# Block products that accumulate on banks copied in between, and the activation's slope in the first pass

## The chip, the cores and the metric

One core of a Trainium2 chip. The time is the device time of one execution in microseconds (us); of the kernel before there are three runs, with a median of 1401.9 us.

## The reference

Three layers on 4608 rows of 512 numbers: an attention block, a mixture of 8 experts, and the layer that this change is about:

```python
def _moe2_ref(x, w_in, w_out, alpha):          # x (4608, 512), w_in (512, 2048), w_out (2048, 512)
    h = x @ w_in
    g = np.maximum(h, 0.0) + alpha * np.minimum(h, 0.0)   # one alpha for each of the 2048 columns
    return (g @ w_out).astype(np.float32)
```

All is fp32. The kernel makes an fp32 product of three matmuls: each operand is split into a rounded high part and the rest, and high x high, high x low and low x high are added up.

## The kernel before

Attention and experts run until about 652 us; the change doesn't touch them. They leave the rows in DRAM. Then comes the last stage, in two passes.

**First pass** (`h = x @ w_in`, stored as `acts` in DRAM). The rows are worked in 8 groups `g` (B = 8) of 544 rows (TB = 544, two halves of TH = 272). The weights stay in SBUF; the output columns are worked in 8 blocks `c` (NP = 8), each of 128 columns in the lower half and 128 in the upper. So there are 64 blocks, numbered n = 8 g + c. Each block is a 2x2 product of halves (columns, rows, and the 512 that are summed over), and it is made with seven products instead of eight, as Winograd's form of Strassen's scheme has it. With U2 = P1 + P6 and U3 = U2 + P7 the four parts are

```
C11 = P1 + P2      C12 = U2 + P5 + P3      C21 = U3 + P4      C22 = U3 + P5
```

Here C11 and C12 go to the lower columns (h = 0 in the buffer `gb`), C21 and C22 to the upper ones (h = 1). A product is 6 matmuls of 128x272 (two halves of the sum, three matmuls each) and has a PSUM bank of its own (`ps_p`). TensorE runs them in the order P1, P2, P6, P7, P4, P5, P3 (`group`, `product`, lines 1558 to 1575), and before each it waits until the bank is free from the block before (line 1566). ScalarE copies P1 to SBUF (`copy_p1`, L897); VectorE does all sums (`add`, L1230, and one wide add for C21 and C22, L1256). SyncE stores both halves of `gb` to `acts` (`store_acts`, L524); `gb` has two buffers, and their first writers wait for the store of two blocks before (`free_acts`).

The moving operands of the seven products of a group are made from the rows `yz`, which SyncE loads in four quarters, one ahead of the stores of each of the blocks 0 to 3 of the group before (`load_y`, L518 and L519). VectorE transposes them (`turn_y`, L1206, in two parts in blocks 4 and 5), makes four sums (`sums_12`, `sums_34`, in blocks 5 and 6), ScalarE rounds the seven (`high`, L889) and VectorE makes the rests (`low`, L1224), both in block 7. The order of the instructions on each engine is written out by hand; every engine takes its own in that order.

In the last group ScalarE and VectorE also split two blocks of w_out per block (L909 and L1279), and the first tile of the second pass is prepared.

**Second pass** (`g @ w_out`), 34 tiles of 128 rows: SyncE loads a tile of `acts` (1 MB, L531), VectorE makes min(h, 0) x alpha (`negative`, L1291) and adds max(h, 0) (`rectify`, L1297), ScalarE rounds (`tile_high`, L917), VectorE makes the rest (`tile_low`, L1302), and TensorE does 48 matmuls of 128x512 (`down`). Tile 0 follows the first pass at once; the first matmul of tile 1 waits for its rest. ScalarE copies the result out (L934) and SyncE stores it.

## Time and profile before

| | us |
|---|---|
| three runs | 1401.13, 1401.9, 1403.9 |
| profiled execution | 1401.62 |
| its span | 1399.8 |
| TensorE busy | 1340.9 (96%) |
| VectorE busy | 824.1 (59%) |
| ScalarE busy | 427.2 (31%) |
| first pass | 669 to 1013.7 |
| second pass | 1013.7 to 1395.5 |

The span is the time from the first to the last instruction; what lies around it is 1.8 us. Busy shares are means over stages that differ much. In the rows below, a releaser in brackets is what ended the idle time of the engine before the instruction. The recorded end of a matmul lies behind the start of the next, since they are pipelined. A row with x2 merges two instructions, and its length runs from the start of the first to the end of the second.

### The profile page before, as it was taken

What the parts mean: (1) busy time and instruction counts of PE and PEld (TensorE: products, weight loads), DVE (VectorE), ACT (ScalarE), POOL (GpSimd) and SP (SyncE); (2) the same over time, 40 slices, a digit from 0 to 9 for tenths busy, and PEclk for the clock granted to TensorE, in tenths of its full rate; (3) what the DMA queues carried; (4) which work ended last, traced back from release to release, by engine and by line L of the source; (5) the groups of instructions that cost most, each with busy time, mean ns of one, the idle gap of its engine ahead of it and who ended that gap; (6) DMA issues with size and microseconds to landing.
All of it is one profiled execution on the core that took longest, in us unless ns stands there. A gap on an engine that the chain in (4) does not pass through costs nothing.

```text
span 1399.8 us, 22413 instructions
## 1 busy us (share of the span) xinstructions
PE 1340.9 (96%) x7807; PEld 1157.3 (83%) x7808; DVE 824.1 (59%) x1065; ACT 427.2 (31%) x625; POOL 186.7 (13%) x232
## 2 busy tenths in 40 slices
PE   8998599999979999997899999999999999999998
PEld 7887478888868888885899999999978888888886
DVE  5677552223555535255677767778875665666652
ACT  6887341111434313134121202212322222222221
POOL 5664022121222222222000000000000000000000
PEclk9999799999989999998899999999999999999999
DMA  8785262112557423452633334433444444444452
GB/s 309 264 265 177 78 240 73 45 43 76 189 176 233 154 103 130 165 159 68 216 126 131 120 135 143 138 125 124 152 122 120 118 124 125 113 112 112 112 120 53
DMA packets 180849, 195.50 MB, mean 140 GB/s; under 512 B 25296, under 2 KB 130768, under 8 KB 180176
## 3 DMA queue, kind: packets, MB, share of 16 engines
q1 hardware_dynamic: 173552, 174.61, 39.5%
q0 software_dynamic: 6112, 19.93, 4.1%
q10 hardware_dynamic: 1152, 0.56, 0.2%
q8 instruction: 16, 0.26, 0.1%
q14 instruction: 17, 0.14, 0.0%
HBM read 127.16 MB, written 67.37 MB: 139 GB/s over the span
## 4 chain that ended last, share of the span: by engine, by line
PE 92%; DVE 3%; ACT 2%; issue 1%; ACTq 0%; DVEq 0%; DMA 0%; POOL 0%; POOLq 0%
PE ps_p L365 13%; PE ps_p L367 13%; PE ps_p L366 13%; PE ps_y L365 5%; PE ps_y L367 5%; PE ps_y L366 5%; PE ps_h L365 5%; PE ps_h L367 5%; PE ps_h L366 5%; PE ps_o L365 5%; PE ps_o L366 5%; PE ps_o L367 5%; PE ps_hT L1511 2%; PE ps_sr L1389 2%; PE ps_xT L1505 1%
## 5 line engine op out<-in xcount | busy, mean ns | idle before, releaser
L365 PE MATMUL ps_p<-b_hi,w_hi 128*128 128x272 f32 x896 | 259.6, 290 | 3.5 <-DVE b_lo L1224 3.5
L366 PE MATMUL ps_p<-b_lo,w_hi 128*128 128x272 f32 x896 | 259.8, 290 | 0.0
L367 PE MATMUL ps_p<-b_hi,w_lo 128*128 128x272 f32 x896 | 259.7, 290 | 0.0
L365 PEld LDWEIGHTS ps_p<-b_hi,w_hi 128*128 128x128 f32 x896 | 169.9, 190 | 4.4 <-DVE b_lo L1224 4.4
L367 PEld LDWEIGHTS ps_p<-b_hi,w_lo 128*128 128x128 f32 x896 | 170.1, 190 | 0.0
L366 PEld LDWEIGHTS ps_p<-b_lo,w_hi 128*128 128x128 f32 x896 | 169.5, 189 | 0.0
L365 PE MATMUL ps_h<-w_hi,xgT_hi 128*128 128x512 f32 x296 | 121.9, 412 | 9.6 <-DVE w_lo L953 7.7
L1144 DVE COPY hid<-ps_h 128x512 f32<-128x512 f32 x74 | 51.1, 691 | 135.6 <-PE ps_h L367 129.4
L365 PE MATMUL ps_y<-w_hi,hidT_hi 128*128 128x512 f32 x296 | 122.7, 414 | 0.0
L1146 DVE SCALAR_TENSOR_TENSOR hidT_lo<-ps_hT,hidT_hi 128x512 fp32r<-128x512 f32 x74 | 51.1, 691 | 121.2 <-ACT hidT_hi L829 119.6
L829 ACT ACTIVATE hidT_hi<-ps_hT 128x512 fp32r<-128x512 f32 x74 | 44.2, 598 | 245.5 <-PE ps_hT L1511 245.5
L367 PE MATMUL ps_h<-w_hi,xgT_lo 128*128 128x512 f32 x296 | 118.0, 399 | 0.0
L1291 DVE SCALAR_TENSOR_TENSOR neg<-gt,alpha 128x2048 f32<-128x2048 f32 x33 | 75.6, 2291 | 71.5 <-DMA gt<-acts 71.5
L366 PE MATMUL ps_h<-w_lo,xgT_hi 128*128 128x512 f32 x296 | 117.7, 398 | 0.0
L367 PE MATMUL ps_y<-w_hi,hidT_lo 128*128 128x512 f32 x296 | 116.5, 394 | 0.0
L1302 DVE TENSOR_TENSOR g_lo<-gt,g_hi 128x2048 fp32r<-128x2048 f32 x34 | 77.9, 2292 | 65.5 <-ACT g_hi L917 65.5
L366 PE MATMUL ps_y<-w_lo,hidT_hi 128*128 128x512 f32 x296 | 116.3, 393 | 0.0
L365 PE MATMUL ps_p<-w_hi,g_hi 128*128 128x512 f32 x272 | 107.5, 395 | 1.3 <-issue 1.3
L367 PE MATMUL ps_o<-w_hi,g_lo 128*128 128x512 f32 x272 | 107.4, 395 | 0.0
L366 PE MATMUL ps_o<-w_lo,g_hi 128*128 128x512 f32 x272 | 107.4, 395 | 0.0
L365 PE MATMUL ps_o<-w_hi,g_hi 128*128 128x512 f32 x272 | 107.4, 395 | 0.0
L366 PE MATMUL ps_p<-w_lo,g_hi 128*128 128x512 f32 x272 | 107.4, 395 | 0.0
(219 smaller groups left out, 2411.6 us busy)
## 6 DMA issues: line engine op xcount, KB each, us to landing
acts<-gb SPq DMA_DIRECT2D x128, 272.0 KB, 2.1
stage<-in_moe_w SPq DMA_DIRECT2D x32, 1024.0 KB, 5.4
gt<-acts SPq DMA_DIRECT2D x32, 1024.0 KB, 6.1
xs_all<-in_xT SPq DMA_DIRECT2D x8, 1024.0 KB, 6.4
xN_all<-in_xN SPq DMA_DIRECT2D x8, 1024.0 KB, 6.3
rows_x<-xrow SPq DMA_DIRECT2D x32, 256.0 KB, 2.6
out_rows<-orow SPq DMA_DIRECT2D x32, 256.0 KB, 2.0
yz<-rows_y SPq DMA_DIRECT2D x30, 256.0 KB, 3.1
```

Of the source, the lines that this page charges most:

```text
L365: pe.matmul(out, s_hi, m_hi, start=start, stop=False)
L366: pe.matmul(out, s_hi, m_lo, start=False, stop=False)
L367: return pe.matmul(out, s_lo, m_hi, start=False, stop=stop)
L829: act.activation(hidT_hi[:, c, :, :], ps_hT[c][:], ACT.Relu).then_inc(hT_hi_ready, 1)
L1144: dve.tensor_copy(hid[:, c, :], ps_h[c][:]).then_inc(h_copied, 1)
L1146: dve.scalar_tensor_tensor(out=hidT_lo[:, c, :, :], in0=ps_hT[c][:], scalar=0.0, in1=hidT_hi[:, c, :, :].bitcast(F32), op0=ALU.max, op1=AL ...
L1291: dve.scalar_tensor_tensor(out=neg[:], in0=gt[k % 2][:], scalar=0.0, in1=alpha[:].unsqueeze(2).to_broadcast([P, KFF, P]), op0=ALU.min, op1 ...
L1302: dve.tensor_tensor(g_lo[k % 2][:], gt[k % 2][:], g_hi[k % 2][:].bitcast(F32), ALU.subtract)\
L1389: mm = pe.matmul(ps_sr[0:NS, h * D:(h + 1) * D], a2T[:, h // GH, cc, (h % GH) * NS:(h % GH + 1) * NS], xN[par][:, cc, h * D:(h + 1) * D], ...
L1505: mm = pe.transpose(ps_xT[:, k, :], xg[:, k * P:(k + 1) * P], ident[:])
L1511: mm = pe.transpose(ps_hT[c][:, k, :], hid[:, c, k * P:(k + 1) * P], ident[:])
```

## The change

The seven products get three pairs of banks by the parity of the block. P1 goes to `ps_a`; when ScalarE has copied it out, P6 is accumulated on the same bank, which then holds U2; that is copied, P7 is accumulated (U3), that is copied, and P4 is accumulated (C21), which ScalarE copies to `gb`. P5 goes to `ps_c`; VectorE makes C22 of it and the copy of U3, then P3 is accumulated on it, and VectorE makes C12 of it and the copy of U2. P2 goes to `ps_b`. TensorE's order is P6, P5, the next block's P2, P7, the next block's P1, P4, P3, and it waits for p1_copied ahead of P6, u2_copied ahead of P7, u3_copied ahead of P4, and c22_ready ahead of P3.

The slope moves from the second pass to the first. h with a slope is h + (1 - alpha) x relu(-h): ScalarE writes relu(-h) of one half of `gb` (128x544) to the one buffer `below`, VectorE multiplies by 1 - alpha (a scalar per partition) and adds to `gb`; first h = 1, then h = 0. The stores wait for that. The second pass rounds the loaded tile directly. The transposes move from blocks 4 and 5 to blocks 2 and 3, the sums to 4 and 5, and ScalarE's roundings are spread over blocks 6 and 7. `load_y` and its place stay. The diff, cut to its core (renamed semaphores, the second pass's arguments and the removed functions are left out):

```diff
@@ order of the products, and of their blocks in w_in (SLOT; b_of is permuted to match)
-P1, P2, P6, P7, P4, P5, P3 = range(7)
+P2, P1, P6, P5, P7, P4, P3 = range(7)
@@ tensors: neg_first and neg_ go; one [P, TB] buffer comes
-        neg_first = sb("neg_first", [P, KFF, P], c=under)
+        below = sb("below", [P, TB], c=under)
-        neg_ = sb("neg", [P, KFF, P], c=sd)
-        ps_pp = pb("ps_p", [P, 7, DM], c=pd)
-        ps_p = [ps_pp[:, i, 0:TH] for i in range(7)]
-        ps_o = [pb("ps_o0", [P, DM], c=pd)[:], ps_pp[:, P1, :]]
+        ps_a = [pb(f"ps_a{i}", [P, DM], c=pd)[:, 0:TH] for i in range(2)]
+        ps_b = [pb(f"ps_b{i}", [P, DM], c=pd)[:, 0:TH] for i in range(2)]
+        ps_c = [pb(f"ps_c{i}", [P, DM], c=pd)[:, 0:TH] for i in range(2)]
+        ps_o = [pb(f"ps_o{i}", [P, DM], c=pd)[:] for i in range(2)]
@@ SyncE, store_acts
-                    wait_apart(sp, (c12_ready, c22_ready)[h], g * NP + c + 1)
+                    wait_apart(sp, acts_ready[h], g * NP + c + 1)
@@ ScalarE
+            def negative(g, c, h):
+                n = NP * g + c
+                act.wait_ge((c12_ready, c22_ready)[h], n + 1)
+                if h:
+                    act.wait_ge(c21_copied, n + 1)
+                    if not (isinstance(n, int) and n == 0):
+                        act.wait_ge(acts_ready[0], n)
+                else:
+                    act.wait_ge(acts_ready[1], n + 1)
+                act.activation(below[:], gb[c % 2][:, h, :], ACT.Relu, scale=-1.0).then_inc(below_ready[h], 1)
+
             def group(g, last=False):
                 for c in range(NP):
-                    copy_p1(g, c)
-                    if c == NP - 1 and not last:
-                        for product in range(7):
-                            high(g + 1, product)
+                    n, par = NP * g + c, c % 2
+                    again = not (isinstance(n, int) and n == 0)
+                    ahead = c >= NP - 2 and not last
+                    act.wait_ge(product_ready[P6], n + 1)
+                    if again:
+                        act.wait_ge(c12_ready, n)
+                    act.activation(part[1][:], ps_a[par], ACT.Copy).then_inc(u2_copied, 1)
+                    if ahead and c == NP - 1:
+                        high(g + 1, P6)
+                        high(g + 1, P5)
+                    act.wait_ge(product_ready[P7], n + 1)
+                    if again:
+                        act.wait_ge(c22_ready, n)
+                    act.activation(part[2][:], ps_a[par], ACT.Copy).then_inc(u3_copied, 1)
+                    if c < NP - 1:
+                        copy_p1(g, c + 1)
+                    elif not last:
+                        copy_p1(g + 1, 0)
+                    act.wait_ge(product_ready[P4], n + 1)
+                    free_acts(act, 1, NP // 2 * g + c // 2, par)
+                    act.activation(gb[par][:, 1, 0:TH], ps_a[par], ACT.Copy).then_inc(c21_copied, 1)
+                    if ahead and c == NP - 2:
+                        high(g + 1, P2)
+                        high(g + 1, P1)
+                    if ahead and c == NP - 1:
+                        high(g + 1, P7)
+                        high(g + 1, P4)
+                    negative(g, c, 1)
+                    negative(g, c, 0)
+                    if ahead and c == NP - 1:
+                        high(g + 1, P3)
                     if last:
                         act.wait_ge(wo_loaded, 64)
-                        act.wait_ge(product_ready[P4], NP * g + c + 1)
                         for f in (c, NP + c):
                             act.activation(w_out(w_hi, f), raw_out(f), ACT.Copy).then_inc(wo_hi_ready, 1)
-                        if c == 5:
-                            tile_high(0, 0)
+                        if c == 6:
+                            tile_high(0, 0, 1)
...
             for product in range(7):
                 high(0, product)
+            copy_p1(0, 0)
@@ VectorE (the adds U2, U3 and the wide C21/C22 go, with negative and rectify)
+            def c11(g, c):
+                free_acts(dve, 0, NP // 2 * g + c // 2, c % 2)
+                add(gb[c % 2][:, 0, 0:TH], ps_b[c % 2], P2, NP * g + c, part[0], p1_copied, c11_ready)
+
+            def slope(g, c, h):
+                dve.wait_ge(below_ready[h], NP * g + c + 1)
+                if h == 0:
+                    dve.wait_ge(c11_ready, NP * g + c + 1)
+                dve.scalar_tensor_tensor(out=gb[c % 2][:, h, :], in0=below[:], scalar=alpha[:, h * NP + c:h * NP + c + 1],
+                                         in1=gb[c % 2][:, h, :], op0=ALU.mult, op1=ALU.add).then_inc(acts_ready[h], 1)
+
             def group(g, last=False):
                 for c in range(NP):
                     n, par = NP * g + c, c % 2
                     ahead = c == NP - 1 and not last
+                    if c == NP - 1 and not last:
+                        low(g + 1, P2)
+                        low(g + 1, P1)
                     if ahead:
                         low(g + 1, P6)
+                    free_acts(dve, 1, NP // 2 * g + c // 2, par)
+                    add(gb[par][:, 1, TH:TB], ps_c[par], P5, n, part[2], u3_copied, c22_ready)
+                    if ahead:
+                        low(g + 1, P5)
+                    if c < NP - 1:
+                        c11(g, c + 1)
+                    elif not last:
+                        c11(g + 1, 0)
+                    add(gb[par][:, 0, TH:TB], ps_c[par], P3, n, part[1], u2_copied, c12_ready)
                     if ahead:
                         low(g + 1, P7)
                         low(g + 1, P4)
+                    slope(g, c, 1)
+                    slope(g, c, 0)
                     if not last:
+                        if c == 2:
+                            turn_y(g + 1, 0, 9)
+                        if c == 3:
+                            turn_y(g + 1, 9, 17)
                         if c == 4:
-                            turn_y(g + 1, 0, 9)
+                            sums_12(g + 1)
                         if c == 5:
-                            turn_y(g + 1, 9, 17)
-                            sums_12(g + 1)
-                        if c == 6:
                             sums_34(g + 1)
+                        if ahead:
+                            low(g + 1, P3)
...
+            dve.tensor_scalar(alpha[:], alpha[:], -1.0, 1.0, ALU.mult, ALU.add).then_inc(beta_ready, 1)
@@ TensorE
+            banks = {P1: ps_a, P2: ps_b, P6: ps_a, P5: ps_c, P7: ps_a, P4: ps_a, P3: ps_c}
...
+                fresh = p in (P1, P2, P5)
                 for k in range(2):
+                    out, m_hi, m_lo = banks[p][c % 2], b_hi[p][:, k, :], b_lo[p][:, k, :]
...
+                    pe.matmul(out, s_hi, m_hi, start=fresh and k == 0, stop=False, skip_group_check=more)
...
+            def first(g, c):
+                free(c21_copied, NP * g + c - 1)
+                product(P1, g, c)
+
+            def second(g, c):
+                free(c11_ready, NP * g + c - 1)
+                product(P2, g, c)
+
+            def group(g, last=False):
                 for c in range(NP):
-                    for p in range(7):
-                        product(p, g, c)
+                    n = NP * g + c
+                    pe.wait_ge(p1_copied, n + 1)
+                    product(P6, g, c)
+                    free(c12_ready, n - 1)
+                    product(P5, g, c)
+                    if c < NP - 1:
+                        second(g, c + 1)
+                    elif not last:
+                        second(g + 1, 0)
+                    pe.wait_ge(u2_copied, n + 1)
+                    product(P7, g, c)
+                    if c < NP - 1:
+                        first(g, c + 1)
+                    elif not last:
+                        first(g + 1, 0)
+                    pe.wait_ge(u3_copied, n + 1)
+                    product(P4, g, c)
+                    pe.wait_ge(c22_ready, n + 1)
+                    product(P3, g, c)
...
+            second(0, 0)
+            first(0, 0)
             group(0)
-            with pe.Fori(1, B) as g:
+            with pe.Fori(1, B - 1) as g:
                 group(g)
+            group(B - 1, last=True)
             down(0, 0, fresh=True)
-            pe.wait_ge(p1_copied, B * NP)
```

## Rows read from the trace of the kernel before

**Rows 1.** Busy time by stretch: PE, PEld, DVE, ACT, POOL, then clock, DMA, GB/s.

```profile
800.00:900.00 100.00, 100.00 (x798) 100.00 (x797) 74.73 (x147) 18.78 (x37) 0.00 (x0) 1.00 0.39 134
...
1100.00:1200.00 100.00, 100.00 (x430) 80.36 (x429) 61.88 (x27) 23.45 (x18) 0.00 (x0) 1.00 0.42 115
```

**Rows 2.** Timeline (start, length, instruction, idle before): the eviction behind P5, two blocks.

```profile
864.71 0.72 DVE L1256 TENSOR_TENSOR gb<-ps_p,part 128x544 f32<-128x544 f32 x1 [1.07 <-PE ps_p L367]
...
869.99 0.72 DVE L1256 TENSOR_TENSOR gb<-ps_p,part 128x544 f32<-128x544 f32 x1 [1.07 <-PE ps_p L367]
```

**Rows 3.** Timeline where P1 and P2 end; 866.68 is P6's first matmul.

```profile
866.12 0.40 ACT L897 ACTIVATE part<-ps_p 128x272 f32<-128x272 f32 x1 [4.88 <-PE ps_p L367]
...
866.68 0.29 PE L365 MATMUL ps_p<-b_hi,w_hi 128*128 128x272 f32 x1
...
866.95 0.44 DVE L1230 TENSOR_TENSOR gb<-ps_p,part 128x272 f32<-128x272 f32 x1 [0.69 <-PE ps_p L367]
```

**Rows 4.** Timeline of the first wait of TensorE in the first pass.

```profile
671.00 0.66 ACT L889 ACTIVATE b_hi<-yz 128x544 fp32r<-128x544 f32 x1 [2.56 <-DVE yz L1215]
...
671.69 0.72 DVE L1224 TENSOR_TENSOR b_lo<-yz,b_hi 128x544 fp32r<-128x544 f32 x1 [0.72 <-ACT b_hi L889]
...
672.47 0.39 PE L365 MATMUL ps_p<-b_hi,w_hi 128*128 128x272 f32 x1 [1.72 <-DVE b_lo L1224]
...
672.70 0.29 PE L366 MATMUL ps_p<-b_lo,w_hi 128*128 128x272 f32 x1
```

**Rows 5.** Timeline of ScalarE and VectorE where instructions follow in a row.

```profile
924.49 1.20 ACT L889 ACTIVATE b_hi<-yT 128x544 fp32r<-128x544 f32 x2
...
925.67 0.43 DVE L1230 TENSOR_TENSOR gb<-ps_p,part 128x272 f32<-128x272 f32 x1
926.02 0.43 DVE L1230 TENSOR_TENSOR part<-ps_p,part 128x272 f32<-128x272 f32 x1
...
929.25 1.34 DVE L1224 TENSOR_TENSOR b_lo<-yz,b_hi 128x544 fp32r<-128x544 f32 x2
...
985.35 1.16 ACT L909 ACTIVATE w_hi<-stage 128x512 fp32r<-128x512 f32 x2 [2.67 <-PE ps_p L367]
...
1002.70 1.92 ACT L917 ACTIVATE g_hi<-gt 128x2048 fp32r<-128x2048 f32 x1 [0.34 <-DVE gt L1297]
1004.52 0.37 ACT L897 ACTIVATE part<-ps_p 128x272 f32<-128x272 f32 x1
```

**Rows 6.** Groups of VectorE instructions: count, busy us, mean ns, idle before.

```profile
L992 DVE TENSOR_SCALAR a<-a,cinv 128x512 f32<-128x512 f32 x16 | 12.0, 791 | 0.3
...
L1279 DVE TENSOR_TENSOR w_lo<-stage,w_hi 128x512 fp32r<-128x512 f32 x14 | 9.0, 682 | 0.0
```

**Rows 7.** Timeline of the pass's first block: P7's start, ScalarE's copy, the pace's return.

```profile
674.55 0.60 PE L365 MATMUL ps_p<-b_hi,w_hi 128*128 128x272 f32 x1 [1.07 <-DVE b_lo L1224]
...
675.37 0.37 ACT L897 ACTIVATE part<-ps_p 128x272 f32<-128x272 f32 x1
...
680.61 0.33 PE L367 MATMUL ps_p<-b_hi,w_lo 128*128 128x272 f32 x1
```

**Rows 8.** Timeline around a y load, its line's landing, and a transpose.

```profile
860.54 0.44 DVE L1230 TENSOR_TENSOR gb<-ps_p,gb 128x272 f32<-128x272 f32 x1
...
862.29 0.41 SPq L519 DMA_DIRECT2D yz<-rows_y  x1
...
DMA to landing us min/median/max: 2.7/2.8/5.5
...
913.70 1.37 DVE L1206 STREAM_TRANSPOSE yT<-yz 128x1152 f32<-128x1152 f32 x1
```

**Rows 9.** Timeline where the second pass goes from tile 0 to tile 1.

```profile
1023.30 2.30 DVE L1302 TENSOR_TENSOR g_lo<-gt,g_hi 128x2048 fp32r<-128x2048 f32 x1 [2.04 <-ACT g_hi L917]
...
1025.70 0.47 PE L365 MATMUL ps_p<-w_hi,g_hi 128*128 128x512 f32 x1 [1.32 <-issue]
```

**Rows 10.** TensorE's busy time and granted clock in a stretch of the attention stage.

```profile
148.00:150.00 2.00, 1.30 (x11) 1.00 0.53 168
```

More of the change, by code:

```diff
@@ L52 @@
 TH = TB // 2
[L53 to L54 removed]
+P2, P1, P6, P5, P7, P4, P3 = range(7)
+SLOT = (1, 0, 4, 5, 2, 3, 6)
 XE = GH * D + E
@@ L1317, in _ @@
             group(B - 1, last=True)
[L1318 to L1324 removed]
+            tile_low(1, 1)
+            with dve.Fori(0, B) as g:
                 for k in range(4):
[L1326 to L1328 removed]
+                    tile_low(4 * g + k + 2, k)
         @block.tensor
```

109 lines of the change are left out of this document (34 added, 75 removed).

## The prediction

> **What bounds the kernel now.** I read the stretches by stage first. In the last stage's first pass (about 669 to 1013.6 us) TensorE is busy 100% of a stretch at clock 1.00, VectorE 75% and ScalarE 19% [rows 1]; the second pass shows TensorE at 100% as well, VectorE at 62%. Then I read the timeline of one block: the eviction that waits for P5 recurs every 5.28 us [rows 2]. A block is 7 products of 6 matmuls, so a product takes 0.754 us and a matmul starts each 0.1257 us, with no hole between products. So no wait is late in the steady state, and faster evictions can't shorten either pass. What is not TensorE at full pace is little: two holes at the start of the pass with a half-rate stretch behind them [rows 7], and one hole between tiles 0 and 1 of the second pass [rows 9].
>
> **Hand-overs, from rows.** ScalarE starts a copy 0.20 us after the next product has begun (P2 began one product before 866.68, at 865.92; the copy starts 866.12) and takes 0.40 us; VectorE starts 0.27 us after (866.95 against 866.68) [rows 3]. A late wait costs TensorE 0.06 us of hop (672.41 to 672.47) and 0.10 us of refill (the second matmul comes 0.23 instead of 0.126 us later) [rows 4]: a product is late by release + 0.16 us minus its due start. On ScalarE a queued instruction starts 0.10 us before the recorded end of the one ahead (1004.52 against 1002.70 + 1.92); two of 128x544 take 1.20 us, so 0.65 us one and 0.55 us each in a row. On VectorE an add takes 0.44 us and 0.35 us in a row; two of 128x544 take 1.34 us, so 0.71 us one and 0.64 us in a row [rows 5]. A hop between the two engines is 0.03 us (671.00 + 0.66 to 671.69) [rows 4].
>
> The new slope has a per-partition scalar, which no 128x544 row shows. Bounds: 0.71 us [rows 5], and 0.11 us more, which L992 (0.791 us, such a scalar) has over a plain 128x512 (0.682) [rows 5, 6]: 0.82 us. I take 0.78 us (0.70 in a row).
>
> **The change, part by part.** I set time 0 at the start of P6 of a block. The new order puts P6 at 0, P5 at 0.75, the next block's P2 at 1.51, P7 at 2.26, the next P1 at 3.02, P4 at 3.77, P3 at 4.52, and the next P6 at 5.28. Matmuls and their operands are unchanged in number and shape, so by themselves they cost nothing more.
>
> (a) *Short chain in every block.* P3 of the block before ends at 0: its add starts 0.27, slope h=1 0.62 to 1.40, ScalarE's negative h=0 (it waits for that slope, since there is one `below`) 1.43 to 2.09. The copy of P6's sum is queued behind it: 1.98 to 2.35, though P6 was finished at 0.75. P7 can start at 2.51 instead of 2.26: 0.25 us late (0.19 with the short slope, 0.29 with the long). P4's wait on the copy of P7's sum is late by 0.60 + 0.16 - 0.75 = 0.01 us; P3's wait for its bank has 0.2 us to spare. Six blocks of each of the first seven groups pay it: 42 x 0.25 = 10.5, and 63 x 0.01 = 0.6. **11.1 us.**
>
> (b) *turn_y moves from block 4 to block 2.* The SyncE queue, which the change leaves as it is, issues the last quarter of the next y in the step of block 3, behind both stores of block 2, and these now wait for the slopes. Slope h=0 of block 2 ends at 2.12 + 0.78 = 2.90. From such a release to the issue of the last load takes 1.31 us (add ends 860.98, issue 862.29), and landing 2.8 us [rows 8]: 7.01. VectorE stands in turn_y until then, transposes (1.37 us, the next can start 1.29 later, by the overlap of rows 5) [rows 8], and only then makes C22 of block 3: 8.33 to 8.77. P3 of block 3 starts at 8.93 instead of 4.78: 4.15 us, 7 groups. Before, two blocks lay between. **29.1 us.**
>
> (c) *P2 of the next group is issued inside block 7*, due at 1.51, and needs its b_lo. ScalarE rounds P2 and P1 in block 6, between the copy of C21 and the negatives: copy -0.55, rounds -0.25 and 0.30, negative 0.85 to 1.51; slope 1.54 to 2.32; negative h=0 2.35 to 3.01; slope h=0 3.04; low P2 on VectorE behind it 3.74 to 4.45. P2 starts 4.61: 3.10 us late, 7 groups. Before, the lows stood ahead of adds that had a block of slack. **21.7 us.**
>
> (d) *Block 0 of the next group.* In block 7 ScalarE rounds P7 and P4 ahead of the negatives and P3 behind, VectorE has lows P7 and P4 ahead of the slopes: add 0.27, lows 0.62 and 1.26, slope 1.90 to 2.68, negative 2.71, round P3 3.26, copy 3.81 to 4.18, P7 at 4.34 instead of 2.26: 2.08 us, 7 groups. **14.6 us.**
>
> (e) *Last group.* Two rounds of w_out (1.16 us the pair, so 0.53 us each in the queue [rows 5]) stand between the negative and the next copy: 0.25 + 1.06 = 1.31 us, six times. Before the last block comes also the first tile's g_hi (1.92, 1.82 in the queue [rows 5]), and no P2 of a next block fills in: 1.31 + 1.82 + 0.75 = 3.88; no P1 covers the wait of P4: 0.76. **12.5 us.**
>
> (f) *Start.* P6 waits for p1_copied, which ScalarE makes after all seven rounds: before, that copy ran 675.37 to 675.74 [rows 7], so P6 starts near 675.8, 5.2 us after P2 and P1. Before, P6 started 672.47 and P7 674.55: the second product ended near 670.60 (the hole before 672.47 less the tail of a matmul), so 1.87 and 1.22 us were lost, and a refill. **+2.0 us.** The half rate after it is paid in both.
>
> (g) *Slopes out of the second pass.* It takes two passes over each of 34 tiles off VectorE, work that lies beside a TensorE without a hole [rows 1], so it is worth nothing, but for one place: tile 1 waits for g_lo until 1025.60, where its turn was 1.3 us earlier, and a refill follows [rows 9]. **-1.6 us.**
>
> Sum of (a) to (g): +89.4 us, with the short slope about 85, with the long 92 (every chain above has one or two slopes).
>
> (h) *Clock.* After holes of 1.72 [rows 4] and 1.07 us, 0.9 us of work between them, 26 matmuls took from 674.55 to 680.61, 0.23 us each where 0.126 is the pace: the clock was at its lower level, 1.2 instead of 2.4 GHz, for 6.1 us [rows 7]. With TensorE 65% busy over 2 us the granted clock stayed 1.00 [rows 10]. That cost 6.06 - 26 x 0.126 = 2.8 us, 2.7 without the refill; 0.2 of it hides a wait of (a). The hole of (b) is longer than those two together: 7 x 2.5 = 17.5. That of (c), 3.1 us, I take at two thirds of that: 12; the last group's 3.9 + 0.8 once: 2.5. That of (d) at nothing. **+32 us**, between 0 and about 60 (three falls per group, 22 x 2.7).
>
> The profiled execution took 1401.6 us (the median of the runs is 1401.9, so it stands for them). 1401.6 + 89.4 + 32 = 1523.0.
>
> The Trainium skill, "TensorE: Matmul & The Clock Gate", section "HAM oscillation", has it that a wait of TensorE long enough to count as idle brings the half clock back each time, and that the work behind it starts cold. Here the start of the pass agrees. By that rule each of (b), (c) and the last group falls every time, for about 37 us instead of 32. The same page, section "A second HAM failure mode", tells of short idles between groups of matmuls on cycled PSUM banks that make the clock swing; that would be the sixth case below.
>
> **The rivals.**
> 1. No fall of the clock: 1401.6 + 89 = 1491 (1484 to 1496). For it: no row shows one hole of 4 us between stretches of dense work. Against it: two smaller holes sufficed. 0.15.
> 2. One of the long waits is covered after all (the y wait, if the loads land or are issued sooner, -29 and its clock; or the lows): 1523 - 29 - 17 = 1477 (1455 to 1482). 0.12.
> 3. More holes than I count: the h=0 bank of gb is free only when the store of two blocks ago has landed (2.0 to 5.8 us), and VectorE's C11 waits for it ahead of the chain of (a), with some 0.3 us to spare; and the clock falls at (d) too. 1545 to 1590. 0.10.
> 4. The group ends are covered and only (a), (e) and (f) stay: 1401.6 + 11.1 + 12.5 + 2.0 - 1.6 = 1426. 0.04.
> 5. Not slower: the copies are in time in every block, so every product starts when due (this decides at 0.16 us ahead of its start). Then only tile 1's gain is left: 1401.6 - 1.6 = 1400. For it: steady work of both engines fits a block (VectorE 2.4 us of 5.28). Against it: the add of P3 is followed by three dependent instructions and a copy, 2.35 us, in a gap of 2.1. 0.03.
> 6. The short holes of (a) alone keep the clock down: 2688 matmuls x 0.1 us = 270, with (a) and parts of the group ends hidden behind slower blocks: about 1690. Against it: the stretch of rows 10. 0.01.
>
> **How the numbers follow.** The forecast has the rest, 0.55: 1523. The range takes in rival 1 and half of 2, and the lower part of 3: 1470 to 1558. A measurement of this kernel tells about 0.2% from no change; all cases but 5 lie beyond it on the slow side: slower 0.97, the same 0.015, faster 0.015.
>
> **What would show it.** P3 of block 3 waiting about 4 us for C22, with VectorE idle before the transpose until the y load lands; P2 at each group's end waiting about 3 us for b_lo; P7 waiting 0.2 to 0.3 us for the copy in other blocks and 2 us in block 0; steady blocks of 5.54 us; the second pass at the old pitch without its hole; PEclk under 1 in the first pass. I am wrong if blocks last 5.28 us, if the transposes start without a wait, or if the time beyond the holes is not at half clock.

## The result and the profile after

The changed kernel takes 1535.1 us (median of 4 runs, 1531.4 to 1536.4), the kernel before 1401.8 us on the same chip: 1.0942 times as long, 95% interval 1.0927 to 1.0957. The forecast was 1523.0, in a range of 1470 to 1558. The profiled execution took 1536.4 us with a span of 1534.6.

By the starts of the matmuls, the first pass begins at 673.4 us (before: 669.0), the second at 1149.2 (1013.0), and the span ends at 1534.6 (1399.8). So of the 134.8 us more, 4.4 come ahead of the pass, 131.8 in it, and the second pass is 1.4 shorter.

Busy time by stretch in the changed kernel answers to [rows 1]; the columns are the same. The first line is most of the first pass, the second lies in the second pass.

```profile
740.00:1140.00 400.00, 333.08 (x2305) 321.04 (x2304) 217.77 (x367) 182.07 (x385) 0.00 (x0) 0.91 0.28 99
1200.00:1300.00 100.00, 100.00 (x430) 80.36 (x429) 20.51 (x9) 22.43 (x18) 0.00 (x0) 1.00 0.43 116
```

TensorE stands idle for 67 of these 400 us, and the granted clock (1.00 is full speed, 0.50 half) is 0.91 on average. VectorE, 75% busy before, is busy 54% of the time here although two slopes per block were added: it waits as well. The second pass is full as before, with VectorE at 21% instead of 62%, and no faster for it. The new operations, from the page's groups of instructions (they answer to [rows 6]):

```profile
L1283 DVE SCALAR_TENSOR_TENSOR gb<-below,alpha,gb 128x544 f32<-128x544 f32 x128 | 100.2, 783 | 57.3 <-ACT below L911 56.9
L911 ACT ACTIVATE below<-gb 128x544 f32<-128x544 f32 x128 | 84.1, 657 | 103.6 <-DVE gb L1283 75.3
```

Who waited for whom in the first pass: engine, line, releaser, us in all, times, the longest. TensorE's three long lines are the copy of U2 ahead of P7 (`ps_a`), C22 ahead of P3 (`ps_c`) and a rest (`b_lo`) ahead of P2 (`ps_b`). The list counts a wait from the recorded end of the matmul ahead, which lies behind the next one's turn, so it misses short ones: by the starts of the matmuls P7 is late 49 times and by 37.9 us in sum.

```profile
DVE gb L1283 <- ACT below L911: 56.9, 71, 1.0
...
DVE gb L1272 <- DMA acts<-gb: 32.7, 33, 2.4
...
DVE yT L1247 <- DMA yz<-rows_y: 30.0, 7, 4.5
...
PE ps_a L1596 <- ACT part L921: 28.7, 27, 3.7
...
PE ps_c L1596 <- DVE gb L1272: 28.0, 7, 4.2
...
PE ps_b L1596 <- DVE b_lo L1265: 21.5, 8, 3.0
```

The chains themselves, from the timeline (start, length, instruction, idle before). First block 3 of a group: the transpose waits for the load of y, C22 follows it, and P3 (the last line) follows C22.

```profile
826.84 1.38 DVE L1247 STREAM_TRANSPOSE yT<-yz 128x1152 f32<-128x1152 f32 x1 [4.31 <-DMA yz<-rows_y]
828.14 0.40 DVE L1272 TENSOR_TENSOR gb<-ps_c,part 128x272 f32<-128x272 f32 x1
...
828.60 0.59 PE L1596 MATMUL ps_c<-b_hi,w_hi 128*128 128x272 f32 x1 [4.03 <-DVE gb L1272]
```

Then block 7 and the next block 0. The slope at 792.50 stands ahead of the rest that P2 needs, and P2 starts at 793.97. At 803.67 P7 of block 0 starts, 0.51 us after the start of the copy of P6's sum.

```profile
792.50 0.78 DVE L1283 SCALAR_TENSOR_TENSOR gb<-below,alpha,gb 128x544 f32<-128x544 f32 x1 [0.78 <-ACT below L911]
...
793.20 1.35 DVE L1265 TENSOR_TENSOR b_lo<-yT,b_hi 128x544 fp32r<-128x544 f32 x2
...
793.97 0.40 PE L1596 MATMUL ps_b<-b_hi,w_hi 128*128 128x272 f32 x1 [2.97 <-DVE b_lo L1265]
...
803.16 0.38 ACT L921 ACTIVATE part<-ps_a 128x272 f32<-128x272 f32 x1
...
803.67 0.39 PE L1596 MATMUL ps_a<-b_hi,w_hi 128*128 128x272 f32 x1 [1.90 <-ACT part L921]
```

And the short chain of an ordinary block: add C12, slope, `below`, the copy, and P7 at 754.91 where 754.66 was its turn (P2 began at 753.91).

```profile
752.70 0.43 DVE L1272 TENSOR_TENSOR gb<-ps_c,part 128x272 f32<-128x272 f32 x1
753.04 0.78 DVE L1283 SCALAR_TENSOR_TENSOR gb<-below,alpha,gb 128x544 f32<-128x544 f32 x1
753.91 0.66 ACT L911 ACTIVATE below<-gb 128x544 f32<-128x544 f32 x1 [0.92 <-DVE gb L1283]
...
754.48 0.38 ACT L921 ACTIVATE part<-ps_a 128x272 f32<-128x272 f32 x1
...
754.91 0.40 PE L1596 MATMUL ps_a<-b_hi,w_hi 128*128 128x272 f32 x1
```

The clock, in stretches of 2 us around the holes of P2 (793.97) and P7 (803.67); a hole is a time in which TensorE waits, and the last column but two is the granted clock. Behind each of these two holes some 3.4 us are at the lower level of 1.2 GHz.

```profile
792.00:794.00 2.00, 0.03 (x1) 0.03 (x1) 1.50 (x3) 1.84 (x4) 0.00 (x0) 1.00 0.35 139
794.00:796.00 2.00, 2.00 (x11) 2.00 (x12) 1.19 (x2) 0.00 (x0) 0.00 (x0) 0.63 0.37 139
796.00:798.00 2.00, 2.00 (x11) 2.00 (x11) 0.79 (x2) 0.40 (x1) 0.00 (x0) 0.52 0.00 0
...
804.00:806.00 2.00, 2.00 (x14) 2.00 (x13) 0.61 (x2) 0.47 (x2) 0.00 (x0) 0.69 0.39 142
806.00:808.00 2.00, 2.00 (x11) 2.00 (x11) 0.44 (x1) 0.86 (x3) 0.00 (x0) 0.50 0.48 136
808.00:810.00 2.00, 2.00 (x17) 2.00 (x17) 1.13 (x2) 0.78 (x2) 0.00 (x0) 0.96 0.00 0
```

The pace shows it directly. Matmuls start 0.23 us apart from 804.77 to 808.17, and 0.13 us apart from there on, so 15 of them took 3.4 us where 1.9 was due: 1.5 us lost.

```profile
807.95 0.39 PE L1597 MATMUL ps_c<-b_lo,w_hi 128*128 128x272 f32 x1
808.17 0.29 PE L1598 MATMUL ps_c<-b_hi,w_lo 128*128 128x272 f32 x1
808.30 0.29 PE L1596 MATMUL ps_a<-b_hi,w_hi 128*128 128x272 f32 x1
```

### The profile page after: what moved, and what is told of

It reads as the page before. It is cut to its first block, busy times and chain, and to the rows that moved or that the text cites. A ratio compares the mean times of both kernels' runs of the same rounds, so it can differ in the third digit from the quotient of the medians.

```text
span 1534.6 us, 22819 instructions
## 1 busy us (share of the span) xinstructions
PE 1396.6 (91%) x7807; PEld 1198.3 (78%) x7808; DVE 673.3 (44%) x934; ACT 570.7 (37%) x945; POOL 186.7 (12%) x232
## 4 chain that ended last, share of the span: by engine, by line
PE 76%; DVE 9%; ACT 6%; issue 4%; DMA 4%; SPq 1%; ACTq 1%; DVEq 0%; POOL 0%; POOLq 0%
PE ps_o L367 8%; PE ps_o L368 8%; PE ps_o L369 8%; PE ps_h L367 4%; PE ps_y L367 4%; PE ps_y L369 4%; PE ps_y L368 4%; PE ps_h L369 4%; PE ps_h L368 4%; DVE gb L1283 4%; PE ps_a L1596 3%; PE ps_a L1598 3%; PE ps_a L1597 3%; DMA acts<-gb 2%; PE ps_hT L1537 2%
## 5 line engine op out<-in xcount | busy, mean ns | idle before, releaser
L367 PE MATMUL ps_o<-w_hi,g_hi 128*128 128x512 f32 x544 | 215.0, 395 | 0.0
L368 PE MATMUL ps_o<-w_lo,g_hi 128*128 128x512 f32 x544 | 214.9, 395 | 0.0
L369 PE MATMUL ps_o<-w_hi,g_lo 128*128 128x512 f32 x544 | 214.9, 395 | 0.0
L1596 PE MATMUL ps_a<-b_hi,w_hi 128*128 128x272 f32 x512 | 163.3, 319 | 35.6 <-ACT part L921 28.7
L1598 PE MATMUL ps_a<-b_hi,w_lo 128*128 128x272 f32 x512 | 157.6, 308 | 0.0
L1597 PE MATMUL ps_a<-b_lo,w_hi 128*128 128x272 f32 x512 | 157.5, 308 | 0.0
L1596 PEld LDWEIGHTS ps_a<-b_hi,w_hi 128*128 128x128 f32 x512 | 106.7, 208 | 46.9 <-ACT part L921 28.1
L367 PEld LDWEIGHTS ps_o<-w_hi,g_hi 128*128 128x128 f32 x544 | 102.1, 188 | 25.0
L368 PEld LDWEIGHTS ps_o<-w_lo,g_hi 128*128 128x128 f32 x544 | 102.1, 188 | 24.8
L369 PEld LDWEIGHTS ps_o<-w_hi,g_lo 128*128 128x128 f32 x544 | 102.0, 187 | 25.0
```

The lines of the kernel that those rows point to most:

```text
L367: pe.matmul(out, s_hi, m_hi, start=start, stop=False)
L368: pe.matmul(out, s_hi, m_lo, start=False, stop=False)
L369: return pe.matmul(out, s_lo, m_hi, start=False, stop=stop)
L1596: pe.matmul(out, s_hi, m_hi, start=fresh and k == 0, stop=False, skip_group_check=more)
L1597: pe.matmul(out, s_hi, m_lo, start=False, stop=False, skip_group_check=more)
L1598: mm = pe.matmul(out, s_lo, m_hi, start=False, stop=k == 1, skip_group_check=more)
```

## The experiments

| kernel | what it is | us | ratio to before, 95% interval |
|---|---|---|---|
| e1 | transposes back in blocks 4 and 5 | 1505.1 | 1.0703 to 1.0739 |
| e2 | y loaded in blocks 0 and 1 | 1489.7 | 1.0585 to 1.0631 |
| e3 | copy of U2 ahead of `below` h = 0 | 1508.4 | 1.0724 to 1.0761 |
| e4 | rests P2 and P1 in block 6 | 1509.0 | 1.0738 to 1.0777 |
| e5 | e2 + e3 + e4, roundings earlier | 1450.6 | 1.0327 to 1.0361 |
| e6 | e5 + first copy of P1 early | 1444.5 | 1.0286 to 1.0314 |
| e7 | e2 without any slope | 1406.7 | 1.0011 to 1.0035 |
| e8 | kernel before + slopes | 1462.4 | 1.0412 to 1.0448 |
| e9 | e6, C11 behind the slopes | 1441.0 | 1.0253 to 1.0285 |
| e10 | e9, work for the next group spread | 1436.2 | 1.0221 to 1.0249 |
| e11 | e10, last group eased | 1433.0 | 1.0202 to 1.0230 |
| e12 | e11, VectorE's extra work behind C22 | 1418.7 | 1.0089 to 1.0123 |

The kernel before took 1403.6 to 1404.0 us beside them. e1 to e4 each take one or two terms of the prediction's sum away. "Late" below is what a product's first matmul starts behind its turn.

**e1.** The y wait, from the side of the transposes:

```diff
-                        if c == 2:
+                        if c == 4:
                             turn_y(g + 1, 0, 9)
-                        if c == 3:
+                        if c == 5:
                             turn_y(g + 1, 9, 17)
```

(with `sums_12` and `sums_34` one block later, too)

> The changed kernel with the transposes and sums back in the blocks where they stood before the change (4 and 5, sums in 5 and 6). Theory (separate holes, each with its own cause): the hole of about 4.2 us before P3 of block 3 goes in 7 groups, with its half-clock stretch (1.35 us each and twice 2.4 to 2.6): 7 x 4.2 + 12 = 41 us off; but block 5 now has a transpose of 1.15 us and two sums of 1.4 us behind the slopes, which end at 2.8 of a block, so C22 of block 6 is made at 5.3 instead of 3.85 and P3 of block 6 is about 1.1 us late: 8 us back. 1535 - 33 = 1502 us. Rival (the y load is not what VectorE waits for, or the time comes back at the next wait in line): less than 10 us off, 1525 or more.

Measured 1505.1, 30 us less. No transpose waits for a load any more. P3 still waits for C22 seven times, now in block 6, 1.2 us late each time, since the rest of the transposes and the sums stand ahead of C22 there.

**e2.** The same wait, from the side of the load:

```diff
-                    if c < QB:
-                        load_y(g + 1, (c,))
+                    if c < 2:
+                        load_y(g + 1, (2 * c, 2 * c + 1))
```

> The changed kernel, its transposes left in blocks 2 and 3, but SyncE issues two quarters of y ahead of the stores of block 0 and two ahead of those of block 1, so that the last one doesn't stand behind the stores of block 2. Theory: the hole before P3 of block 3 goes and nothing takes its place: 1535 - 41 = 1494 us. Some us back are possible where a store is late behind two more loads. Rival (the place of the transpose in VectorE's order is the cause, not the load): no gain, 1530 or more.

Measured 1489.7, 45.4 less. P3's line is gone from the list of waits, and 12 half-rate stretches are left of 22. Both edits remove the hole of (b), by different ways. Its price was 29.8 us of holes and 12.3 us at half rate behind them (see below). e1 gets these 42 us back and pays 9 of them again at P3 of block 6 and some 3 at P2 and P7. e2 pays nothing at P3, since its transposes in blocks 2 and 3 find C22 in time, and the half rate came behind only three of its seven holes of (d).

**e3.** The short chain of (a) and (d):

```diff
                     negative(g, c, 1)
+                    if c < NP - 1:
+                        copy_u2(g, c + 1)
+                    elif not last:
+                        copy_u2(g + 1, 0)
                     negative(g, c, 0)
```

> The changed kernel, with ScalarE's copy of U2 of the next block ahead of the negative of h=0 instead of behind it. Theory: this takes the slope of h=1 and the negative out of the way of P7. The waits of P7 in ordinary blocks go (42 x 0.34 = 14 us), the 2.15 us in block 0 of each group with its half-clock stretch (7 x 3.3 = 23 us), and 1.3 us in six blocks of the last group (8 us): 1535 - 45 = 1490 us. P2's 3.1 us and P3's 4.2 us stay. Rival (the copy-and-accumulate chain itself is too long for a block, whatever stands in ScalarE's queue): P7 waits as before, less than 10 us off.

Measured 1508.4, above what was expected. Most of P7's waits went, but P3 waited more. The wait list of e3:

```profile
PE ps_c L1604 <- DVE gb L1280: 38.1, 12, 5.4
...
DVE yT L1255 <- DMA yz<-rows_y: 29.6, 7, 4.4
```

Twelve times and 38.1 us instead of seven and 28.0. TensorE comes to P3 of block 3 sooner, but y doesn't land sooner, so part of the time that (a) and (d) gave back was spent there: this P3 is 5.2 to 5.5 us late instead of 4.0 to 4.4, 8 us more in seven groups. The rest of the 18 us between expected and measured is mostly new short waits: P4 eleven times, 8.5 us in sum (0.8 before the edit), and P3 in other blocks, 5.7 us.

**e4.** The rests ahead of P2:

```diff
-                    if c == NP - 1 and not last:
-                        low(g + 1, P2)
-                        low(g + 1, P1)
...
                     add(gb[par][:, 0, TH:TB], ps_c[par], P3, n, part[1], u2_copied, c12_ready)
+                    if c == NP - 2 and not last:
+                        low(g + 1, P2)
+                        low(g + 1, P1)
```

> The changed kernel, with VectorE's two rests for P2 and P1 of the next group in block 6 ahead of the slopes instead of in block 7. Theory: b_lo of P2 is there at about 1.5 of block 7, so P2's wait of 3.1 us goes; the slopes of block 6 come 1.3 us later, and P7 of block 7, hidden behind P2's hole until now, is 1.5 us late: 7 x 1.6 us off, and some of the half-clock stretches behind P2's hole (1.25 us each): 1535 - 11 - 6 = 1518 us. Rival (P2 waits for something else): no change.

Measured 1509.0, 26 less, where 17 were expected. P2's wait is gone; P7's grew from 28.7 to 36.2 us in sum, since the slopes of block 6 now come later (P7 of block 7 is 1.4 us late, as expected). The 9 us beyond the expectation are in part the clock's: the half rate costs 12 us less than in the changed kernel, not 6, for it came behind only four of the seven holes of (d). The profiled execution also began the pass 4 us earlier.

**e5.** The three together, and the roundings P6, P5 and P3 earlier (`copy_u2` as in e3, loads as in e2, rests as in e4):

```diff
+                    if ahead and c == NP - 2:
+                        high(g + 1, P6)
+                        high(g + 1, P5)
                     if ahead and c == NP - 1:
                         high(g + 1, P3)
+                    negative(g, c, 0)
```

> The changed kernel with all holes between blocks taken on at once: y loads issued in blocks 0 and 1, the copy of U2 ahead of the negative of h=0, the rests of P2 and P1 in block 6, and ScalarE's roundings of P6, P5 (block 6) and P3 (block 7) put between the copy of U2 and that negative, where ScalarE would wait for VectorE's slope. Banks, accumulation and slopes are as changed. Theory (accumulating on copied banks costs nothing by itself; all of the loss was queue order): left are the start (+2 us), the last group (about 4 us before the last block and the first tile) and crumbs of 0.1 us in some blocks (5 us), less 1.6 us for tile 1: 1401.8 + 2 + 4 + 5 - 1.6 = 1411 us. Rival (the chain of product, copy, product is too tight, since P4 has no time to spare, and slips in every block): 64 x 0.3 us or more, 1430 us.

Measured 1450.6, 40 us above the theory. The rival's time fits, its mechanism doesn't: P4 is late in 11 of the 64 blocks, not in every one (10.0 us in sum, 3.2 of it in the last block). Two half-rate stretches are left, at the pass's start and end, so the clock's part is nearly gone. What remains are waits that the longer ones had covered, above all P3's: 43 times, 22.6 us late in sum. The wait list of e5:

```profile
DVE gb L1280 <- DMA acts<-gb: 78.7, 62, 2.5
...
PE ps_c L1604 <- DVE gb L1280: 16.5, 30, 1.0
```

C11 waits in 62 of 64 blocks until the store of two blocks ago has landed, and C12 and the slopes are queued behind it.

**e6.** The start:

```diff
             for product in range(7):
                 high(0, product)
-            copy_p1(0, 0)
+                if product == P1:
+                    copy_p1(0, 0)
```

> As e5_waits_out, and ScalarE copies P1 of the very first block right after it has rounded P1, instead of after all seven. Theory: P6 no longer waits 5.3 us at the start, only for its own b_lo (1.9 us), and P5 and P2 of the next block fill in before P7: 3 us less than e5_waits_out, and no half-clock stretch there (2 us): 1406 us, between the kernel before and e5_waits_out. Rival (the products at the start wait for their b_lo one after the other anyway): the same as e5_waits_out within 1 us.

Measured 1444.5, 6.1 less where 5 were expected. The hole ahead of P6 shrank from 5.3 to 2.0 us, and the half-rate stretch behind it from 21 slow matmuls to 14, 0.8 us less. By the starts of the matmuls the pass is 3.7 us shorter (390.7 to 387.0); the rest of the 6.2 us between the two profiled executions lies ahead of the pass, which began 2.5 us earlier and varies in all kernels (see below).

**e7.** What the accumulation on copied banks costs alone. This is e2 with `below` and the slopes left out altogether, so negative numbers of h pass unchanged; stores wait for the adds and copies:

```diff
-                    wait_apart(sp, acts_ready[h], g * NP + c + 1)
+                    wait_apart(sp, (c12_ready, c22_ready)[h], g * NP + c + 1)
+                    if h:
+                        wait_apart(sp, c21_copied, g * NP + c + 1)
+                    else:
+                        wait_apart(sp, c11_ready, g * NP + c + 1)
...
-                    negative(g, c, 1)
-                    negative(g, c, 0)
...
-                    slope(g, c, 1)
-                    slope(g, c, 0)
```

> The changed kernel with y loads in blocks 0 and 1 and with the activation's slope left out altogether (neither the negatives nor the multiply-adds; the second pass rounds h itself). The copies, the accumulation on the banks and the queue order are as changed. Theory: without slopes no wait of a block is late; left are the start (+2 us), 2.5 us before the last block, less 1.6 us: about 1405 us. Rival (the accumulation on copied banks is what costs): P7's and P4's waits stay, 1440 us or more.

Measured 1406.7. The wait list of e7, TensorE's lines in the first pass with the hole of the start and two small ones:

```profile
PE ps_a L1596 <- ACT part L903: 5.1, 1, 5.1
...
PE ps_a L1596 <- ACT part L925: 1.2, 1, 1.2
...
PE ps_b L1596 <- DVE b_lo L1267: 0.7, 1, 0.7
```

So the four times per block that TensorE goes on with a bank which another engine has read in between (P6, P7, P4 and P3) cost it nothing in the steady state. Beside e2, which has the same loads, the slopes cost 83 of its 86 us. No run without slopes has the loads of the changed kernel; that the wait for y hangs on the slopes too, through the stores that wait for them, is argued and not shown.

**e8.** The other half alone: the kernel before, with both slopes at the end of each block, the stores waiting for them, and the second pass without the activation:

```diff
-                    wait_apart(sp, (c12_ready, c22_ready)[h], g * NP + c + 1)
+                    wait_apart(sp, acts_ready[h], g * NP + c + 1)
...
                     add(gb[par][:, 0, TH:TB], P3, n, gb[par][:, 0, TH:TB], c12_ready)
+                    slope(g, c, 1)
+                    slope(g, c, 0)
```

> The kernel before (seven banks, its own order of products and its sums on VectorE), with only the slope moved into the first pass as the change has it (ScalarE's negative, VectorE's multiply-add, stores behind them). Theory: banks have a block of slack, so no chain is late, but VectorE has about 9.7 us free in a group of 42.2 and the slopes want 16 x 0.70 = 11.2: TensorE slips 1.5 us in each of 7 groups and some 4 us in the last, less 1.6 us: 1415 us. Rival (a hidden engine stays hidden): 1400 us. Other rival (the slopes cost TensorE as much as in the changed kernel): 1480 us or more.

Measured 1462.4, 47 above my sum. VectorE in two blocks of e8:

```profile
792.00 0.78 DVE L1249 SCALAR_TENSOR_TENSOR gb<-below,alpha,gb 128x544 f32<-128x544 f32 x1
793.57 0.79 DVE L1249 SCALAR_TENSOR_TENSOR gb<-below,alpha,gb 128x544 f32<-128x544 f32 x1 [0.79 <-ACT below L908]
794.27 0.44 DVE L1243 TENSOR_TENSOR gb<-ps_p,part 128x272 f32<-128x272 f32 x1
...
796.67 0.44 DVE L1243 TENSOR_TENSOR gb<-ps_p,gb 128x272 f32<-128x272 f32 x1
797.03 0.78 DVE L1249 SCALAR_TENSOR_TENSOR gb<-below,alpha,gb 128x544 f32<-128x544 f32 x1
```

The block repeats after 5.03 us (792.00 to 797.03) and VectorE waits only for `below`, 0.79 us between the two slopes; my sum of busy times had left that out. Eight such blocks and the work for the next group take 49.5 us a group by the repeat of the groups, where TensorE needs 42.2. With VectorE doing all seven sums, the slope makes it the bound. In the changed kernel the banks and ScalarE have taken over some of the sums (VectorE is 54% busy in the stretch above), and e12 below shows that what is left is nearly all order.

**e9.** Against the store wait of e5:

```diff
-                    if c < NP - 1:
-                        c11(g, c + 1)
-                    elif not last:
-                        c11(g + 1, 0)
                     add(gb[par][:, 0, TH:TB], ps_c[par], P3, n, part[1], u2_copied, c12_ready)
...
                     slope(g, c, 0)
+                    if c < NP - 1:
+                        c11(g, c + 1)
+                    elif not last:
+                        c11(g + 1, 0)
```

> e6_start_too with one move: VectorE makes C11 of the next block behind both slopes instead of ahead of C12, so that its wait for the landed store of two blocks ago no longer holds up C12. Theory (what e5 and e6 still lose is that wait: it takes about 2.5 us from a slope's end to the landed store, and C12, both slopes and ScalarE's negative stand behind it): VectorE's waits for that store go, P3 and P7 are in time in ordinary blocks, and about 1.3 us stay late in blocks 7 and 0 of each group, where C11 now stands ahead of C22 and of rests: 1401.8 + 20 + 4 - 1.6 = 1424 us. Rival (VectorE has too little time for its work in a block, whatever the order): no gain, 1440 us or more.

Measured 1441.0, only 3.5 under e6. The line of the store wait is gone from the list, and P3's wait rose from 16.5 us in e5 to this:

```profile
PE ps_c L1605 <- DVE gb L1281: 20.7, 42, 0.9
```

The store wait was real but not what decided, and the 1424 us expected were missed by 17. P4's waits fell (9.7 us late in e6, 3.0 here), but P3 is now late 49 times, 29.4 us in sum, in the blocks 0 and 3 to 7: C22 came late for another reason. The time is the rival's (1440 or more), but its reason, too little time on VectorE, is refuted by e12, which does the same work in 1418.7. Those short waits had no fall of the clock behind them, as this stretch of e9 shows (columns as before):

```profile
700.00:1000.00 300.00, 282.39 (x2162) 273.54 (x2160) 197.67 (x341) 169.68 (x354) 0.00 (x0) 1.00 0.33 117
```

**e10.** Two things spread over blocks 6 and 7 instead of in a heap: ScalarE's roundings, and VectorE's rests and C11 of the next group ahead of C12 of block 7:

```diff
+                    if ahead and c == NP - 2:
+                        high(g + 1, P2)
...
+                    if ahead and c == NP - 1:
+                        high(g + 1, P7)
...
+                    if ahead:
+                        c11(g + 1, 0)
+                        low(g + 1, P7)
```

> e9_c11_behind with the work for the next group spread so that each piece stands in a gap: ScalarE rounds P2 before the copy of U3 and P1 before the copy of C21 of block 6, P6 ahead of and P5 behind the negative of h=0, P7 behind the copy of U3 and P4 behind C21 in block 7; VectorE makes the rests of P2 and P1 ahead of C12 of block 6 and C11 of the next group ahead of C12 of block 7. Theory: block 6 to 7 without a wait, about 0.5 us late in block 0 (7 x 0.5), 5 us in the last group, start 1.5 us better than in the kernel before, less 1.6 us: 1401.8 + 3.5 + 5 - 1.5 - 1.6 = 1407 us. Rival (crumbs of refills and copies add up to 0.2 us a block): 1418 us.

Measured 1436.2, above both the theory (1407) and the rival (1418). Only blocks 1 and 2 of a group are free of waits. VectorE there, C12 at 783.21 and again at 788.48, which is 5.27 us and the old period:

```profile
783.21 0.44 DVE L1284 TENSOR_TENSOR gb<-ps_c,part 128x272 f32<-128x272 f32 x1 [1.29 <-PE ps_c L1610]
...
785.90 0.43 DVE L1284 TENSOR_TENSOR gb<-ps_b,part 128x272 f32<-128x272 f32 x1
786.74 0.44 DVE L1284 TENSOR_TENSOR gb<-ps_c,part 128x272 f32<-128x272 f32 x1 [0.41 <-ACT part L930]
788.48 0.44 DVE L1284 TENSOR_TENSOR gb<-ps_c,part 128x272 f32<-128x272 f32 x1 [1.29 <-PE ps_c L1610]
...
793.35 0.40 PE L1608 MATMUL ps_c<-b_hi,w_hi 128*128 128x272 f32 x1 [0.40 <-DVE gb L1284]
```

The last line is P3 of block 3, in which a transpose stood ahead of C22. By its start it is 0.6 us late, and P3 of the blocks 0 and 3 to 7, where rests, transposes or sums stand ahead of C22, is late by 0.1 to 0.7 us in the first seven groups: with the last group, 49 times and 21.1 us in sum. In the bracket of 788.48 lies what points to e12: VectorE is idle for 1.29 us between C22 and C12. It waits there in 50 of the 64 blocks, and has only 0.41 ahead of C22.

**e11.** The last group: a block of w_out less in block 5, where the first tile is rounded instead:

```diff
-                        if c == 6:
+                        if c == 5:
                             tile_high(0, 0, 1)
+                        else:
+                            round_out(c if c < 5 else c - 1)
```

> e10_spread with the last group eased: the first tile's high part is made in block 5 in place of two rounds of w_out, which move one block on each (the last pair behind the group), and its rest behind C22 of the last block. Theory: the 3.9 us before P7 and P3 of the last block become 0.6 + 0.8, and the second pass starts about 1 us late: 2 us less than e10_spread, 1405 us. Rival (the second pass waits for the moved w_out parts): 1 to 3 us more than e10_spread.

(the rest of that tile moves behind C22 of block 7)

Measured 1433.0, 3.2 under e10. In e10 the rounding of the first tile in front of the last block's copies still made P4 3.0 and P3 1.3 us late, with a half-rate stretch behind; here they are 1.3 and 0.5 us late, P4 of the block before is 0.5, and that stretch is gone.

**e12.** VectorE's transposes, sums and rests of w_out go into that gap, and so does the rest for P6, which stood ahead of C22 (those for P5, P2 and P1 were in the gap already). The rest for P7 moves behind C12 and that for P4 between the slopes; P3's stays at the block's end:

```diff
+                        if 1 <= c < 6:
+                            rest_out(c - 1)
+                        if c == 7:
+                            tile_low(0, 0)
                     add(gb[par][:, 0, TH:TB], ps_c[par], P3, n, part[1], u2_copied, c12_ready)
+                    if ahead:
+                        low(g + 1, P7)
                     slope(g, c, 1)
+                    if ahead:
+                        low(g + 1, P4)
                     slope(g, c, 0)
                     if c < NP - 1:
                         c11(g, c + 1)
+                    if ahead:
+                        low(g + 1, P3)
```

(the transposes and sums stand unchanged, but now ahead of `add(... P3 ...)`, as the first lines do)

> This is e11 with VectorE's transposes of y, its sums, its last roundings (P4, P3, P2, P1) and the rests of w_out in the gap that VectorE has between C22 and C12, instead of ahead of C22; the rounding P4 stands between the two slopes, and C11 of the next group behind C22 of block 7. Theory: what is left in e11 is order ahead of C22 alone, 0.36 to 0.67 us in each of blocks 3 to 6 of seven groups (some 15 us) and some 2.6 us of the last group. Then the median is about 1412 to 1418 us, with some 0.5 us a group left in block 0, the start and the last block. Rival: the work only moves the wait, to P7 (which then waits for C12 or for the slope behind it) or to the next P3: 1428 us and more. Neither expects it below the kernel before.

Measured 1418.7, 14.3 under e11 and 1.0106 of before: most of the theory's drop, just above the 1418 at the upper edge of what was expected. In the first seven groups there is no wait left in blocks 1 to 7 (in the last one P4 waits twice, 0.5 and 1.3 us). One is left at the group's turn, and it is longer than the 0.5 us expected:

```profile
757.91 0.43 DVE L1289 TENSOR_TENSOR gb<-ps_b,part 128x272 f32<-128x272 f32 x1
...
760.47 0.44 DVE L1289 TENSOR_TENSOR gb<-ps_b,part 128x272 f32<-128x272 f32 x1 [1.55 <-DMA acts<-gb]
760.83 1.35 DVE L1282 TENSOR_TENSOR b_lo<-yz,b_hi 128x544 fp32r<-128x544 f32 x2
761.60 0.40 PE L1618 MATMUL ps_a<-b_hi,w_hi 128*128 128x272 f32 x1 [1.43 <-DVE b_lo L1282]
```

C11 of the next group waits for the store of two blocks ago, the rest for P6 stands behind it, and P6 starts 1.6 us late. With its refill (the 0.10 us by which the second matmul comes late) and 0.34 us at the P3 that follows, this comes to 2.0 us in each of seven groups, 14.0 in all, about the whole distance of the first pass from that of the kernel before (358.8 against 344.0 us). To put that rest ahead of C11 is the next edit. It wasn't tried, and if it gave all of this back it would reach the kernel before, not pass it.

## Why the prediction was right

All steps stood but one part of (h): that the hole of (d) has no fall of the clock behind it. Their sizes come from the starts of all 2688 matmuls of the pass in the profiled execution. The pitch is the 0.1257 us from one start to the next; a step is what a product starts late, with the refill of 0.10 us, and (h) is what the matmuls behind lose by a slower pace. The start, (f) and its clock, is the difference to the kernel before.

| step | predicted, us | measured, us |
|---|---|---|
| (a) P7 of ordinary blocks | 11.1 | 15.8 |
| (b) P3 of block 3, y load | 29.1 | 29.8 |
| (c) P2 of the next group | 21.7 | 22.7 |
| (d) P7 of block 0 | 14.6 | 15.0 |
| (e) last group | 12.5 | 13.0 |
| (f) start | 2.0 | 2.1 |
| (g) second pass | -1.6 | -1.4 |
| (h) clock | 32 | 33.3 |
| begin of the pass | 0 | 4.4 |

The measured column sums to 134.7 of the 134.8. Of the 12 us between the forecast of 1523.0 and the median of 1535.1, (a) and the begin of the pass are the most, 4.7 and 4.4.

- **(a)** was mis-sized. Of its 42 waits three are 1.3 to 1.7 us, at which C11 had waited for a store ahead of the chain (rival 3's mechanism, 4.5 us here). Of the others, the seven in block 4 are covered by the hole of (b) and the slow matmuls behind it, and 32 cost 0.35 us on average instead of 0.25. The hop from the slope to `below` is 0.09 us (753.04 + 0.78 to 753.91), where I had 0.03 from [rows 4], and in the chain shown above the copy of P6's sum ends 2.45 us after P6's start at 752.41, where I had 2.35. Blocks with such a wait and nothing else mostly last 5.5 to 5.7 us, where 5.54 was forecast.
- **(b)** e1 and e2 remove it from two sides, and are 30 and 45 us faster. The seven P3 are 4.0 to 4.4 us late for 4.15, by the landing of the load. e3 adds what I had not weighed: this wait is tied to a transfer and not to TensorE, so it takes up any time saved ahead of it.
- **(c), (d), (e)** are right within 1 us each, the clock apart; the slope took 0.783 us where I took 0.78 between bounds of 0.71 and 0.82. e4 confirms (c), and e11 the last block's part of (e).
- **(h)** was right in the sum by errors that cancel, which is luck. I put 2.5 us on each of seven falls at (b), two thirds of that on (c) and nothing on (d). Measured: falls at seven of seven holes of (b), six of seven of (c), and all seven of (d). But most of these stretches last 3.4 us at the granted clock and cost 1.5 (1.2 to 1.5); only two in the groups lasted about as long as that of the kernel before (5.8 and 6.3 us, 2.6 and 2.8). So (b) cost 12.3 instead of 17.5, (c) 9.1 instead of 12, (d) 10.6 instead of 0, the end 1.8 instead of 2.5, and the start 0.5 less than in the kernel before. Taking the price of a fall from the one stretch of [rows 7] was the error, and so was exempting (d). Nor is a fall at (d) sure: behind these holes of 2.0 to 2.1 us it came in six of seven groups of e1, three of e2 and four of e4.
- **Begin of the pass**: it varies between 668.4 and 673.4 us over the profiled executions of all these kernels, in no order that their edits explain (e11 671.0, e12 668.4). The 4.4 us are no effect of the change that I can show.

The Trainium skill, "TensorE: Matmul & The Clock Gate", section "HAM oscillation", lets a long idle bring the half clock each time. This trace agrees for the seven holes of (b), 4.0 to 4.4 us; of the shorter ones it shows the same behind six of seven of 3.1 us and all seven of 2.0 to 2.1, and behind none of the nine of 1.2 to 1.7. The same page's section "A second HAM failure mode" has short idles between banks in turn make the clock swing; no run here shows that: in e9 P3 is late 39 times between 700 and 1000 us, by 0.3 to 1.0 us, and the granted clock there is 1.00.

Of the rivals, that without a fall (1), those with a covered wait (2, 4) and that of no loss (5) are ruled out by the rows above. Of the third two parts came true, the fall at (d) and the store wait, the latter in three blocks only; it became general when the other waits were gone (e5). Rival 5 decides at 0.16 us ahead of each start; e10 meets that in blocks 1 and 2 of a group and e12 in blocks 1 to 7, by order alone.

## What to carry to other kernels

Where TensorE is 100% busy at full clock, moving VectorE's work from one such stage to another has next to nothing to gain (here 1.4 us in the second pass) and much to lose; the best order found ends 1% behind. When a change puts a dependent instruction at the end of a block, walk each in-order queue for what now stands ahead of the instruction that releases TensorE, and put movable work into the gap that begins when TensorE has been released (here between C22 and C12), not ahead of the release. Waits in such a schedule are not additive: e2, e3 and e4 gave 45, 27 and 26 us alone, 98 in sum, but 85 together in e5, which also has three roundings earlier.

## What the runs showed of the hardware that I had not expected

- In the changed kernel all seven holes of 2.0 to 2.1 us had a half-rate stretch behind them, and such stretches were mostly 3.4 us long, not 6: 1.5 us each. The nine holes of 1.2 to 1.7 us had none. But the length of the hole doesn't settle it: of the 28 holes at (d) in the changed kernel, e1, e2 and e4 eight had none, e10's one hole of 2.1 us had none, and neither had two of 3.0 us in e3.
- Accumulating on a bank that another engine has copied out in between has no price on TensorE beyond the wait: e7 ran its ordinary blocks without a hole.
- The hand-over between VectorE and ScalarE on one buffer costs 0.78 to 0.79 us of VectorE's time between two dependent slopes, in the changed kernel and in e8 alike, where nothing else stands between them. It is mostly the length of `below` (0.66) and two hops.
